# Transformer block kernel: three output tiles per token tile in the mixing stage, angles kept in PSUM, low parts of the token weights on VectorE

## The reference

```
def _moe2_ref(x, w_theta, w_tok_r, w_tok_i, w_ch):
    theta = x @ w_theta                       # x: 2 x 768 x 512
    zr, zi = x * cos(theta), x * sin(theta)
    yr = einsum('ts,bsd->btd', w_tok_r, zr)   # w_tok_*: 768 x 768
    yi = einsum('ts,bsd->btd', w_tok_i, zi)
    u = x + yr + yi
    return u + maximum(u @ w_ch, 0.0)         # w_theta, w_ch: 512 x 512
```

## Time and profile before

| | |
|---|---|
| median of 3 runs | 717.95 us |
| profiled execution, whole | 716.68 us |
| its span | 714.9 us |
| mixing stage, its first to its last instruction | 501 us to the end |
| TensorE busy (matmul), whole span | 626.5 us, 88% |
| VectorE / ScalarE / GpSimd busy | 59% / 49% / 41% |

### The profile page before, as it was taken

How to read it: one execution, slowest core, us unless ns; L and a number is a source line. 1 busy time by engine, 2 the same in 40 slices (tenths; PEclk the granted TensorE clock), 3 DMA queues, 4 the chain that set the end, 5 groups by cost and what they waited for, 6 DMA issues and landing times. The chain is left out here.

```text
span 714.9 us, 10319 instructions
## 1 busy us (share of the span) xinstructions
PE 626.5 (88%) x3677; PEld 496.4 (69%) x3678; DVE 418.4 (59%) x706; ACT 349.9 (49%) x524; POOL 292.3 (41%) x202
## 2 busy tenths in 40 slices
PE   3899999999999981089999999997469899699998
PEld 1666766666766651088899989996347688588886
DVE  6677777777777638144655456522598865812212
ACT  4777776767776745043455336511355644522100
POOL 5661725427170003533664356410566447533100
PEclk9999999999999995579999999999698999899999
DMA  9105161533607008776766676211711111222301
GB/s 297 72 1 177 54 228 24 206 102 128 208 22 258 1 1 312 269 257 223 266 210 203 215 260 231 86 62 60 263 62 46 42 45 44 80 68 77 130 29 60
DMA packets 50975, 96.09 MB, mean 134 GB/s; under 512 B 16624, under 2 KB 16624, under 8 KB 50928
## 3 DMA queue, kind: packets, MB, share of 16 engines
q1 hardware_dynamic: 48720, 88.38, 36.3%
q0 software_dynamic: 1920, 6.29, 2.5%
q10 hardware_dynamic: 288, 0.79, 0.3%
HBM read 69.23 MB, written 26.21 MB: 134 GB/s over the span
## 5 line engine op out<-in xcount | busy, mean ns | idle before, releaser
L881 POOL TENSOR_TENSOR w_lo<-stage,w_hi 128x1024 fp32r<-128x1024 f32 x28 | 85.2, 3061 | 85.7 <-ACT w_hi L876 85.7
L365 DVE TENSOR_REDUCE scores<-scores 128x1 f32<-128x768 f32 x96 | 92.8, 966 | 41.8 <-PE scores L480 40.6
L306 ACT COPY probs_t<-turned 128x768 f32<-128x768 f32 x96 | 76.7, 799 | 62.1 <-PE turned L489 61.8
L314 ACT ACTIVATE probs<-scores,bias,scale 128x768 f32<-128x768 f32 x96 | 95.4, 994 | 13.0 <-DVE bias L372 12.5
L489 PE MATMUL turned<-ident,probs 128*128 128x128 f32 x576 | 79.7, 275 | 5.1 <-ACT probs_t L306 5.1
L489 PEld LDWEIGHTS turned<-ident,probs 128*128 128x128 f32 x576 | 67.4, 141 | 14.3 <-issue 11.5
L970 PE MATMUL up<-xt_hi,w_hi 128*128 128x256 f32 x256 | 73.4, 287 | 2.0 <-DVE xt_lo L923 2.0
L970 PE MATMUL up<-xt_hi,w_lo 128*128 128x256 f32 x256 | 73.2, 286 | 0.0
L970 PE MATMUL up<-xt_lo,w_hi 128*128 128x256 f32 x256 | 73.1, 286 | 0.0
L501 PE MATMUL pv<-probs_t,v_in 128*64 128x384 f32 x384 | 72.3, 498 | 0.9 <-ACT probs_t L306 0.9
L480 PE MATMUL scores<-k_aug,q_aug 76*128 76x384 f32 x192 | 60.0, 394 | 7.5 <-DVE k_aug L358 5.1
(11 more groups left out here) (158 smaller groups left out, 1290.7 us busy)
## 6 DMA issues: line engine op xcount, KB each, us to landing
stage<-in_w SPq DMA_DIRECT2D x64, 512.0 KB, 4.9
wt_raw<-in_w_tok SPq DMA_DIRECT2D x12, 768.0 KB, 4.3
x_slots<-zeros SPq DMA_DIRECT2D x7, 1024.0 KB, 8.6
y_slots<-zeros SPq DMA_DIRECT2D x7, 1024.0 KB, 11.2
q_raw<-in_qT SPq DMA_DIRECT2D x16, 384.0 KB, 5.2
k_raw<-in_kT SPq DMA_DIRECT2D x14, 384.0 KB, 5.8
x_in<-x_slots SPq DMA_DIRECT2D x10, 512.0 KB, 5.4
y_slots<-y_out SPq DMA_DIRECT2D x8, 512.0 KB, 2.8
```

Of the source, the lines that this page charges most:

```text
L306: nc.scalar.copy(probs_t[j % 2][:, a, :, t % 3 * P:(t % 3 + 1) * P].rearrange("k (b n) q -> k b n q", b=2), turned[:, :, 0:HALF].rearrange ...
L314: nc.scalar.activation(probs[g % 3][:].rearrange("p (b n) -> p b n", b=2), scores[g % 2][:, :, 0:HALF], ACT.Exp, bias=bias[:, pair, a, t:t ...
L365: nc.vector.tensor_reduce(neg_max[g % 2], scores[g % 2][:, :, 0:HALF], AX.XY, ALU.max, negate=True).then_inc(s_neg, 1)
L881: name.tensor_tensor(w_lo[w][:, r, :], stage[:, r, :], w_hi[w][:, r, :].bitcast(F32), ALU.subtract).then_inc(done, 1)
```

## The change

- Three output tiles (0, 1, 2) instead of two take each token tile as it comes. Output tile n runs n token tiles behind, so `tokens(2)` as a block is gone.
- Steps L1216 and L1219 of `reduce_angle` write back into the `theta` bank; only the clamp writes `angle`. The projection two tiles on waits for `4 * c - 4` steps (all four steps of tile c-2) instead of `4 * c - 6`.
- All low parts of the token weights are made on VectorE. GpSimd keeps the gathers and `times_x`.
- Columns 1, 3 and 5 are loaded into the first three quarters of `w_raw`, the others into `wt_raw`; load i (2 to 6) waits for column i-2. The load of w_ch moves behind load 6 and column 5. From load 7 on there is only `wt_raw`.
- Column i's high and low parts, and the `add_x`, take new places in the lists of ScalarE and VectorE.

The diff, without its unchanged surroundings:

```
@@ -1033,7 +1033,7 @@
-    s_wt = sem("m_wt")
+    s_wt = [sem(f"m_wt{n}") for n in range(2)]
@@ -1060,19 +1060,38 @@
+    def raw_of(i):
+        if i in (1, 3, 5):
+            return 1, w_raw[:].rearrange("p k n -> p (k n)")[:, 0:2 * T * P].rearrange("p (m s t) -> p m s t", m=2, s=T)
+        return 0, wt_raw[:]
+    def landed(i):
+        if i in (1, 3, 5):
+            return 8 * (i + 1)
+        return 16 * (i // 2 + 1) if i <= 6 else 16 * (i - 2)
+    def columns_done(engine, i):
+        engine.wait_ge(s_wtl, i + 1)
-            if i > 0:
-                sp.wait_ge(s_wth, i)
-                sp.wait_ge(s_wtl, i)
-            sp.dma_start(wt_raw[:], w_tok[i % T, :, :, :, :]).then_inc(s_wt, 16)
-        load_wt(0)
-        sp.wait_ge(s_whi, 1)
-        sp.wait_ge(s_wlo, 1)
+            n, buffer = raw_of(i)
+            if i == 1:
+                sp.wait_ge(s_whi, 1)
+                sp.wait_ge(s_wlo, 1)
+            elif i >= 2:
+                columns_done(sp, i - 2 if i <= 6 else i - 1)
+            sp.dma_start(buffer, w_tok[i % T, :, :, :, :]).then_inc(s_wt[n], 16)
+        for i in range(7):
+            load_wt(i)
+        columns_done(sp, 5)
-        for i in range(1, NC):
+        for i in range(7, NC):
@@ -1086,11 +1105,6 @@
-        def columns_low(i):
-            pool.wait_ge(s_wth, i + 1)
-            nc.gpsimd.tensor_tensor(wt_lo[i % 3][:], wt_raw[:], wt_hi[i % 3][:].bitcast(F32),
-                                    ALU.subtract).then_inc(s_wtl, 1)
@@ -1109,12 +1123,6 @@
-            if c in (0, 3):
-                columns_low(1 + c // 3)
-            if 7 <= c <= 9:
-                columns_low(c - 4)
-        for i in range(6, NC):
-            columns_low(i)
@@ -1122,10 +1130,11 @@
-            act.wait_ge(s_wt, 16 * i + 16)
+            n, raw = raw_of(i)
+            act.wait_ge(s_wt[n], landed(i))
-            high(wt_hi[i % 3][:], wt_raw[:], s_wth)
+            high(wt_hi[i % 3][:], raw, s_wth)
@@ -1167,25 +1176,28 @@
+            if c == 0:
+                columns_high(1)
-            if c in (1, 3):
-                columns_high(c // 2 + 1)
-            if c >= 8:
-                columns_high(c - 5)
+            if c == 1:
+                columns_high(2)
+            if c >= 9:
+                columns_high(c - 6)
+        columns_high(6)
-        columns_high(7)
-        columns_high(8)
+        for i in (7, 8, 9):
+            columns_high(i)
-            if n in (1, 3, 5):
-                columns_high(9 + n // 2)
+            if n in (1, 3):
+                columns_high(10 + n // 2)
@@ -1211,19 +1223,23 @@
+            nc.vector.scalar_tensor_tensor(theta[q][:], turns[:], -TWO_PI_HI, theta[q][:], ALU.mult,
+                                           ALU.add).then_inc(s_r, 1)
+            dve.wait_ge(s_r, 4 * c + 2)
+            nc.vector.scalar_tensor_tensor(theta[q][:], turns[:], -TWO_PI_LO, theta[q][:], ALU.mult,
+                                           ALU.add).then_inc(s_r, 1)
+            dve.wait_ge(s_r, 4 * c + 3)
-            nc.vector.scalar_tensor_tensor(angle[q][:], turns[:], -TWO_PI_HI, theta[q][:], ALU.mult,
-                                           ALU.add).then_inc(s_r, 1)
-            dve.wait_ge(s_r, 4 * c + 2)
-            nc.vector.scalar_tensor_tensor(angle[q][:], turns[:], -TWO_PI_LO, angle[q][:], ALU.mult,
-                                           ALU.add).then_inc(s_r, 1)
-            dve.wait_ge(s_r, 4 * c + 3)
-            nc.vector.tensor_scalar(angle[q][:], angle[q][:], BELOW_PI, -BELOW_PI, ALU.min, ALU.max).then_inc(s_r, 1)
+            nc.vector.tensor_scalar(angle[q][:], theta[q][:], BELOW_PI, -BELOW_PI, ALU.min, ALU.max).then_inc(s_r, 1)
+        def columns_low(i):
+            dve.wait_ge(s_wth, i + 1)
+            low(wt_lo[i % 3][:], raw_of(i)[1], wt_hi[i % 3][:], s_wtl)
@@ -1237,28 +1253,31 @@
-        dve.wait_ge(s_wth, 1)
-        low(wt_lo[0][:], wt_raw[:], wt_hi[0][:], s_wtl)
+        columns_low(0)
-            if c == 8:
-                add_x(0)
-                add_x(1)
-                add_x(c - 7)
+                add_x(c - 9)
+            if c in (0, 2):
+                columns_low(1 + c // 2)
+            if c >= 9:
+                columns_low(c - 6)
+        add_x(3)
+        columns_low(6)
-        add_x(5)
-        add_x(6)
+        for n in (4, 5, 6):
+            add_x(n)
+            columns_low(n + 3)
@@ -1268,6 +1287,8 @@
+            if n in (1, 3):
+                columns_low(10 + n // 2)
@@ -1295,14 +1316,14 @@
-                pe.wait_ge(s_r, 4 * c - 6)
+                pe.wait_ge(s_r, 4 * c - 4)
-                if n % T in (0, 1):
+                if n % T == 0:
@@ -1312,7 +1333,7 @@
-            pe.wait_ge(s_wtl, n + 1)
+            columns_done(pe, n)
@@ -1325,7 +1346,7 @@
-                pe.wait_ge(s_r, 4 * NC - 2)
+                pe.wait_ge(s_r, 4 * NC)
@@ -1339,25 +1360,18 @@
-        for s in range(T):
-            if s == 0:
-                pe.wait_ge(s_wtl, 1)
-            from_tile(0, s)
-            if s == 1:
-                pe.wait_ge(s_wtl, 2)
-            if s >= 1:
-                from_tile(1, s - 1)
-            if s < T - 1:
+        for s in range(T + 2):
+            for n in range(3):
+                if s == n:
+                    columns_done(pe, n)
+                if 0 <= s - n < T:
+                    from_tile(n, s - n)
+            if s + 4 < NC - 1:
-        from_tile(1, T - 1)
-        turn_x(10)
-        angles(9)
-        tokens(2)
-        turn_x(11)
-        angles(10)
-        angles(11)
+        angles(NC - 1)
```

## The result

| | before | after |
|---|---|---|
| median (fewest to most) | 718.0 us (717.04 to 718.53, 4 runs) | 701.78 us (701.04 to 702.36, 4 runs) |
| profiled execution, whole | 716.68 us | 702.36 us |
| span | 714.9 us | 700.5 us |

The ratio is 0.9782, with an interval of 0.977 to 0.9794: 16 us faster. The prediction said 706.0, from 702.5 to 711.5; the direction was right, and the size fell just outside the range. The same kernel run again beside later experiments gave 702.43 us and a ratio of 0.9793 (0.9771 to 0.9814).

The account below looks back on a forecast made before the run. TensorE, the busiest engine, was taken to lose 14.3 us to idling and slow clock in the mixing stage. 1.0 lost at the start, 14.3 won, 2.1 lost at the end: -11.2 us, named 706.0, range 702.5 to 711.5.

Parts of the forecast that it names:

- What bounds the kernel: Mixing stage: from projection 4's end to the end of `tokens(7)`, 101.1 us hold 86.8 of TensorE work; 14.3 idle or slow.
- Step 1: `reduce_angle`: angles in PSUM escape the lock with GpSimd, cutting it from 3.9 to 2.6 us, VectorE's tile cycle 7.0 to 5.6.
- bound of 1.4: VectorE writing to PSUM: upper limit in us for one operation, twice the 0.70 of one that reads it.
- the rival that hung on it: Slow PSUM writes in `reduce_angle` eat the gain at 1.7 us a write; about 721 us total at x = 1.2; chance 0.07.
- Step 2: Token tiles: three units make TensorE's share 7.3 us against VectorE's 5.6, so from tile 5 on TensorE waits for nothing.
- Step 3: Stage start: two low parts on VectorE delay projection 4 by 1.0 us; slow clock kept, so the projection takes 5.26.
- Step 4: Middle, after projection 4 to the end of `tokens(7)`: 86.8 us of work run without waits, 14.3 us won.
- Step 5: Ahead of the first channel projection: late w_ch and loads 7 to 9 delay `x_low(12)` to 630.4 instead of 628.3, 2.1 us lost.
- The sum: Whole kernel: 1.0 - 14.3 + 2.1 = -11.2 us, giving 705.5 from the profiled execution or 706.8 from the median; named 706.0.
- mark (b): Start of the first channel projection, counted from the mixing stage's first transposition; 134.4 us in the kernel before.
- the clock stays: Rival: the clock stays at 2.4 GHz through projection 4, saving 2.5 us, about 703.5 us total; chance 0.2.
- three signs of being wrong: L1216 over 1 us; TensorE waiting for z_lo, wt_lo or x_low between 545 and 625; last gap over 6 us.

Follow-up runs that it names:

- e2: The changed kernel with the angles back in the SBUF tile `angle` (and the old wait counts), the rest kept: 709.97 us.
- e11: e2 run once more, unchanged: 709.72 us (707.78 to 710.4).
- e4: The kernel before the change with only the angles put in PSUM: 710.94 us.
- e1: The changed kernel with two output tiles instead of three taking the token tiles as they come, the rest kept: 702.29 us.
- e3: The changed kernel with the low parts of columns 1 to 11 back on GpSimd, both raw buffers, three units and angles in PSUM kept: 711.64 us.
- e9: The changed kernel with all columns loaded into wt_raw, each after the low part before it, and w_ch loaded early into w_raw: 712.5 us.
- e10: The changed kernel itself run once more: 702.43 us, ratio 0.9793 to the kernel before.
- e5: The changed kernel with one more 128x512 subtraction on VectorE (part of column 2's low part made twice) ahead of columns_low(2): 703.73 us.
- e6: The changed kernel with the whole of column 2's low part made twice on VectorE ahead of columns_low(2): 704.9 us.
- e8: e7 with x_high and x_low of tiles 12 and 13 moved ahead of column 9, in front of the channel stage: 694.46 us.
- e7: The changed kernel with the high and low parts of columns 1 and 2 moved later, out of the early chain: 696.55 us.

## Why the prediction was right or wrong

**What bounds the kernel** was read rightly: 14.3 us of idle time and slow clock between projection 4 and the end of `tokens(7)`. After the change that stretch holds 86.8 us of work and takes 86.9, counted as there: from 539.64 to 626.54, where the idle time of 0.45 begins. The trace shows no wait of TensorE in it.

**Step 1, the angles in PSUM: right.** A write to PSUM costs what the read does: 696 and 695 ns (taken: 0.70), the clamp 691 ns (taken: 0.69). Its bound of 1.4 and the rival that hung on it are out. (That rival's sum has a slip: 8 (2x - 1.7) is 16x - 13.6, not 13.4; it still breaks even near x = 1.0.) e2, e11 and e4 show its worth from both sides: 7 to 8 us with the rest of the change, 7 without it.

**Step 2, three units: right in its numbers, wrong in its reason.** I wrote that TensorE's share becomes 7.3 us, "more than VectorE's 5.6", and that so TensorE waits for nothing. The 5.9 of two units is more than 5.6 too, and e1 shows that this was enough. With both numbers on the page I still credited the third unit with the gain.

**Step 3, the low parts on VectorE: here is the step that failed,** the slow clock of projection 4. Its start was nearly right: projection 4 starts 0.5 us later from the stage's start (28.5 against 28.0), not 1.0. The larger error is the clock: "I take the slow clock of before: the projection takes 5.26 and ends at 541.5". It took 2.83 by the same count. The clock did fall early in the stage, but under projection 2, after an idle time of 2.78 us, where it cost nothing: TensorE would have waited for `x_low(3)` anyway. I took the likeness of two idle times, 3.3 and 3.81, for proof; what ran ahead of them was not alike. The timeline of TensorE in the kernel before shows 2.1 us of work between an idle time of 1.66 and the one of 3.81:

```profile
529.38 0.47 PE L1308 MATMUL y<-z_hi,wt_hi 128*128 128x512 f32 x1 [1.66 <-DVE z_lo L1193]
...
530.85 0.60 PE L1278 MATMUL m_tp<-ident,x_tok 128*128 128x128 f32 x4
```

In the changed kernel it is 9.8 us of work without a gap:

```profile
523.96 0.47 PE L1310 MATMUL theta<-wm_hi,m_xt_hi 128*128 128x512 f32 x1 [2.78 <-DVE m_xt_lo L1205]
...
533.18 0.60 PE L1299 MATMUL m_tp<-ident,x_tok 128*128 128x128 f32 x4
...
536.81 0.47 PE L1310 MATMUL theta<-wm_hi,m_xt_hi 128*128 128x512 f32 x1 [3.04 <-DVE m_xt_lo L1205]
```

That this difference is the reason fits e3 (short pieces of work between gaps of 1.07, 1.18 and 0.92, then 2.56), and e9 better still: the same idle time as in e1 and e10, 3.01 us, but only 4.8 us of work ahead of it, and the slow clock was there from the first matmul.

```profile
534.41 0.47 PE L1303 MATMUL theta<-wm_hi,m_xt_hi 128*128 128x512 f32 x1 [1.14 <-DVE m_xt_lo L1198]
...
542.21 0.70 PE L1303 MATMUL theta<-wm_hi,m_xt_hi 128*128 128x512 f32 x1 [3.01 <-DVE m_xt_lo L1198]
```

But it is not the whole reason. In e2 9.6 us of work without a gap, followed by 3.74 us of idle time, brought the slow clock at once; in e5 9.9 us and 3.71 brought it only at the sixth matmul.

```profile
535.25 0.77 PE L1310 MATMUL theta<-wm_hi,m_xt_hi 128*128 128x512 f32 x1 [3.74 <-DVE m_xt_lo L1205]
```

So the cause stays open in part; it was not tried by itself. e5 and e6 show how close to its edge the changed kernel runs: 0.7 us more idle time cost 1.6 us of slow clock on top. This step is 2.4 us of the error.

**Step 4, the middle: right,** to 0.1 us. Column 3 was there in time: its low part was done at 580.9, `tokens(3)` began at 582.1, a margin of 1.2 us where I had 7.3 - 5.9 = 1.4. With the angles in SBUF (e2) it was 2.0 us late.

**Step 5, the end of the middle: right in its mechanism, its hole mis-sized:** 2.1 us predicted, 0.45 measured (0.93 in e10). From the end of the last angle projection to `x_low(12)` I had 35.7 us; the chain has 33.9 (593.01 to 626.86). Column 6 was done 10.7 instead of 11.4 us after that projection, load 7 landed 4.0 us after its issue and not 4.9, and loads 8 and 9 took 4.5 and 4.1, none 5.5. The load of w_ch took 5.75 instead of 6.5; VectorE was done with its low part (and one `add_x`) at 609.3, just when column 7's high part was there. In e8, with column 9 moved behind the channel stage's input, the hole is gone, which shows that it was this chain.

**The sum.** Predicted for mark (b): 1.0 - 14.3 + 2.1 = -11.2. Measured: 118.66 - 134.36 = -15.7. The difference of 4.5 is 0.5 (start) + 2.4 (clock) + 1.7 (hole), less 0.1 in the middle. The tail gives back 0.3, since the first channel projection took 3.00 instead of 2.73 after its gap, and the stage started 1.1 us later than in the trace of before: 15.7 - 0.3 - 1.1 = 14.3, the difference of the two profiled executions (the medians differ by 16.2). The rival "the clock stays" was what happened, and at 703.5 it was nearest; it kept the 2.1 us. My range left out just the case in which clock and hole both went, with the words that "both the clock and the 2.1 us would have to go"; taken off the forecast, the two give 706.0 - 2.5 - 2.1 = 701.4, and 701.78 was measured. None of the three signs of being wrong that I had named came: they watched the write to PSUM, waits in the middle and a larger last gap, and none the clock.

What of the change did it, each taken out alone: the angles in PSUM 7 to 8 us (e2, e11), the low parts on VectorE 9 (e3), the second raw buffer, with w_ch early again, 10 (e9), the third unit 0 (e1). They add up to far more than 16; the traces show that the hole before the channel stage grows in all of the first three (1.76, 6.86 and 3.43 us against 0.45), and that projection 4 runs slow in all three. Only the angles were also put into the kernel before by themselves (e4); the low parts and the buffer were not.

**Left open:** which pattern of work and idle time decides that the clock falls at once (e3, 2.56 us), a few matmuls later (e4, e5), or not at all (the changed kernel, 3.04 us). And why the untouched stages end up to 3 us apart.

## What to carry to other kernels

Write down for each engine how long it needs per turn of a pipeline, and compare before giving an edit the credit: what was needed was VectorE below TensorE with some room. 5.6 us against 5.9 was enough (e1); 7.0 against 7.3, reached by giving TensorE a third unit, was not (e2), because low parts of the weights stand on VectorE too. Where two engines share a lock, moving one operand to PSUM can be worth more than the rate that it costs. And once the steady part is fed, look at its two ends: here 5 to 6 us more (e7) lay in work on weights that stood in the lists long before anyone needed it.

## What the runs showed of the hardware

- VectorE writing float32 to PSUM, in place with one operand from SBUF, took 696 ns for 128x512, where the same operation that only reads PSUM took 688 in the mean (L1216 before), and none of the 24 took more than 697 ns, whatever GpSimd did.
- GpSimd gains as well: its product took 1495 ns in the mean before and 1291 with nothing but the angles moved to PSUM (e4); 1375 in e1, and 1552 with the angles in SBUF (e2). The Trainium skill (SBUF — State Buffer, the section on two physically separate sides) tells of an exclusive lock held for a whole instruction; the 2.17 us of the low part at 533.89, against 1.77 alone, agree, as do the 1.31 and 1.40 in e2.
- A load of 768 KB took 4.0 to 4.5 us in the chains in front of the channel stage (5.54 in the kernel before), and 4.8 to 7.8 when it was issued some 5 us after the stage's first transposition, beside the last gathers of rows; the same kernel has 5.4 in one trace and 7.6 in the other.
